# Readers' waits, warming passes and the placing of expert weights in a fused linear attention, soft MoE and gated layer

## The reference

```python
# 1. linear attention with decay; batch 4, heads 8, sequence 768, head size 48
for t in range(S):
    cur = einsum('bhd,bhe->bhde', u[None] * kt, vt)
    y[:, :, t] = einsum('bhd,bhde->bhe', rt, state + cur)
    state = w[None, :, :, None] * state + einsum('bhd,bhe->bhde', kt, vt)
# 2. soft MoE on x of 3072 x 384; 8 experts x 4 slots, hidden 1024
logits = x @ phi
d = softmax over tokens;  slot_input = d.T @ x
h = relu(slot_input[e] @ w1[e]);  slot_out[e] = h @ w2[e]
x = (softmax over slots of logits) @ slot_out
# 3. layer with a gate, d_ff 2048
h = x @ w_in;  g = h * sigmoid(1.702 * h);  out = g @ w_out
```

## Time and profile before

| what | value |
|---|---|
| timed runs, median (lowest to highest) | 395.88 us (395.13 to 398.88) |
| profiled execution: its time | 394.21 us |
| profiled execution: its span | 392.4 us |
| mean granted clock of PE, share of full | 0.982 |
| PE busy | 376.1 us, 96% of the span |
| DVE / ACT / POOL busy | 229.1 / 187.5 / 112.1 us |
| transfers | 63.77 MB, mean 163 GB/s over the span |

### The profile page before, as it was taken

How to read it: one execution, slowest core, us unless ns; L and a number is a source line. 1 busy time by engine, 2 the same in 40 slices (tenths; PEclk the granted TensorE clock), 3 DMA queues, 4 the chain that set the end, 5 groups by cost and what they waited for, 6 DMA issues and landing times.

```text
span 392.4 us, 9064 instructions
## 1 busy us (share of the span) xinstructions
PE 376.1 (96%) x3206; PEld 296.4 (76%) x3206; DVE 229.1 (58%) x419; ACT 187.5 (48%) x432; POOL 112.1 (29%) x125
## 2 busy tenths in 40 slices
PE   4599999999999999899999999999999999999996
PEld 4487787878787444478888888888888888888885
DVE  5477888777885400187665565565565565565561
ACT  1034445555444531376656546544644564555552
POOL 5678987888774020054310000000000000000000
PEclk9579999999999999999999999999999999999999
DMA  7799999999999989930002000200200020002002
GB/s 233 246 364 389 368 381 342 355 345 352 375 326 372 373 287 388 393 121 3 0 0 82 1 0 0 80 0 0 82 0 0 0 80 0 0 0 80 0 2 81
DMA packets 28966, 63.77 MB, mean 163 GB/s; under 512 B 3088, under 2 KB 17056, under 8 KB 28560
## 3 DMA queue, kind: packets, MB, share of 16 engines
q1 hardware_dynamic: 27600, 62.99, 44.4%
q10 hardware_dynamic: 1344, 0.49, 0.7%
HBM read 58.75 MB, written 4.72 MB: 162 GB/s over the span
## 4 chain that ended last, share of the span: by engine, by line
PE 78%; DMA 9%; POOL 5%; SPq 3%; issue 2%; DVE 2%; ACT 0%; DVEq 0%; POOLq 0%
PE bank L592 11%; PE bank L590 11%; PE bank L591 11%; PE pair L590 5%; PE pair L592 5%; PE pair L591 5%; DMA krb<-kr 5%; PE bank L337 4%; PE pair L375 4%; DMA ring<-win 4%; PE bank L577 4%; PE pair L366 3%; PE pair L358 3%; PE bank L396 2%; POOL rkn L1031 2%
## 5 line engine op out<-in xcount | busy, mean ns | idle before, releaser
L813 DVE TENSOR_TENSOR gf<-bank,sg 128x512 f32<-128x512 f32 x72 | 49.7, 692 | 63.4 <-ACT sg L981 63.2
L981 ACT ACTIVATE sg<-bank 128x512 f32<-128x512 f32 x72 | 42.9, 598 | 73.3 <-PE bank L577 73.2
L590 PE MATMUL bank<-glo,whi 128*128 128x512 f32 x192 | 74.7, 389 | 0.0
L592 PE MATMUL bank<-ghi,wlo 128*128 128x512 f32 x192 | 74.7, 389 | 0.0
L591 PE MATMUL bank<-ghi,whi 128*128 128x512 f32 x192 | 74.7, 389 | 0.0
L819 DVE TENSOR_TENSOR glo<-gf,ghi 128x512 fp32r<-128x512 f32 x96 | 69.4, 723 | 0.2
L987 ACT ACTIVATE ghi<-gf 128x512 fp32r<-128x512 f32 x96 | 59.9, 624 | 1.0 <-DVE gf L813 0.9
L591 PEld LDWEIGHTS bank<-ghi,whi 128*128 128x128 f32 x192 | 36.0, 188 | 7.5
L592 PEld LDWEIGHTS bank<-ghi,wlo 128*128 128x128 f32 x192 | 36.0, 188 | 7.5
L590 PEld LDWEIGHTS bank<-glo,whi 128*128 128x128 f32 x192 | 36.0, 188 | 7.5
L861 ACT ACTIVATE yt<-pair 112x512 f32<-112x512 f32 x24 | 14.4, 598 | 56.9 <-PE pair L375 56.9
(11 more groups left out here) (162 smaller groups left out, 520.8 us busy)
## 6 DMA issues: line engine op xcount, KB each, us to landing
ring<-w SPq DMA_DIRECT2D x24, 512.0 KB, 6.2
rkb<-rk SPq DMA_DIRECT2D x23, 512.0 KB, 5.4
krb<-kr SPq DMA_DIRECT2D x24, 384.0 KB, 5.5
ring<-w SPq DMA_DIRECT2D x4, 1536.0 KB, 14.2
ring<-w SPq DMA_DIRECT2D x8, 768.0 KB, 10.6
vb<-v SPq DMA_DIRECT2D x24, 192.0 KB, 5.4
out<-ob SPq DMA_DIRECT2D x18, 256.0 KB, 2.1
ring<-win SPq DMA_DIRECT2D x3, 1024.0 KB, 14.1
```

Of the source, the lines that this page charges most:

```text
L590: pe.matmul(o, w_hi, lo, start=(f == 0), stop=False)
L592: pe.matmul(o, w_lo, hi, start=False, stop=(f == KF - 1)).then_inc(prod_ps, 1)
L813: dve.tensor_tensor(gf[:, f % 2, :], bank[f % 4][:, :], sg[:, f % 2, :], ALU.mult).then_inc(gf_ok, 1)
L981: act.activation(sg[:, f % 2, :], bank[f % 4][:, :], ACT.Sigmoid, scale=1.702).then_inc(sg_ok, 1)
```

## The change

There are five edits. The warming products at the start become 17 in place of 12, and four more stand behind the turning of `wks`. PE's wait for `phi` moves to the last step of the first chunk (step 3). The waits for the constants and the cleared tiles move to their first readers: on DVE to the first `mask`, on POOL to the multiplication by u (constants) and to the first `vd` (cleared tiles). In the order of work, DVE scales step 1 ahead of masking step 0, and POOL makes `kk` of step 0 ahead of the bonus of step 1. SP loads no w1 in the first chunk, five pieces in each of chunks 1 to 4 (two of them in the last step of a chunk), and four in the last chunk; there are 24 pieces in both kernels.

```diff
-WARM = 12
+WARM = 17
@@ SP, step
-                sp.dma_start(ring_flat[:, bass.ds(n * FE, FE)], w1_v[n]).then_inc(w1_in, 16)
+                if not is_first(c):
+                    for i in (b,) if b < B - 1 or is_last(c) else (b, b + 1):
+                        piece = (B + 1) * (c - 1) + i
+                        sp.dma_start(ring_flat[:, bass.ds(piece * FE, FE)], w1_v[piece]).then_inc(w1_in, 16)
@@ PE, scores and step
                     last.then_inc(wkn_ps, 1)
+                    keep_warm(LG, 4)
...
+                if is_first(c, b - 3):
+                    pe.wait_ge(s_phi, 16 * 5)
...
-            pe.wait_ge(s_phi, 16 * 5)
@@ DVE, ahead of the steps, mask and step
-            dve.wait_ge(zeroed, 5)
-            dve.wait_ge(s_const, 16 * 2)
...
+                if is_first(c, b):
+                    dve.wait_ge(zeroed, 5)
+                    dve.wait_ge(s_const, 16 * 2)
...
-                if not is_first(c, b):
+                if is_first(c, b - 1):
+                    scale(c, b)
                     mask(*prev(c, b))
-                scale(c, b)
+                elif is_first(c, b):
+                    scale(c, b)
+                else:
+                    mask(*prev(c, b))
+                    scale(c, b)
@@ POOL, ahead of the steps, bonus, bonus_values and step
-            pool.wait_ge(s_const, 16 * 2)
-            pool.wait_ge(zeroed, 5)
...
                 pool.wait_ge(rk_ok, n + 1)
+                if is_first(c, b):
+                    pool.wait_ge(s_const, 16 * 2)
...
                 wait(pool, rs_used, n - 1)
+                if is_first(c, b):
+                    pool.wait_ge(zeroed, 5)
...
             def step(c, b):
-                bonus(c, b)
                 if b == 1 and is_first(c):
                     scaled_keys(0, 0)
+                bonus(c, b)
```

## The result

The changed kernel takes 389.28 us (median of four runs, 388.57 to 389.61). The kernel before, timed beside it and in the runs shown ahead, has a median of 396.75 us in four (395.13 to 398.88). The ratio on record is 0.9844, with a 95% interval of 0.981 to 0.9877: faster by 1.2 to 1.9% (the plain ratio of the two medians is 0.981, the interval's lower end). The profiled executions took 394.21 and 389.61 us, 4.6 us apart; the medians are 7.5 us apart.

The account below looks back on a forecast made before the run. PE's work was taken to bound everything from 54 us, moving as a block with its entry to chunk 1. 5.0 us gained there and 0 later gave a median of 390.9 us, range 389.0 to 394.0.

Parts of the forecast that it names:

- The start: Chunk 0 up to scores 4: earlier waits, new order and no w1 bring scores 4 from 31.41 to 26.4, gaining 5.0 us.
- the warming term: PE's start: ten more products at 0.196 us an instruction take 1.96 us more, so warming ends at 9.5.
- more is gained: Rival, chance 0.07: at the start kk begins at 11.4 and another microsecond comes free, giving 389.5 us.
- A clock of 1.00 from 10 to 24 us: Sign to look for in the changed profile: PE's clock stays at full level through the start.
- The rival had the fall: Rival, chance 0.15: PE's clock falls again near 13 us, about 2.1 us reach scores 3, result 393.0 us.
- The step that puts four more warming products behind the turning: PE between 11.2 and 12.8: 8 instructions, 1.0 to 1.6 us, fill idle time before scores 1; cover thin by 0.4.
- So 0 is my value: Fifth w1 piece in chunks 1 to 4: costs 0 us, with ends at 0 and 5.2 us.
- the estimate of 399.4 us: Chunks 1 to 4 at the skill's 341 GB/s: four chunks 8.5 us longer; the prediction held the trace against it.
- The slack of 4.0 us: Seventh vd ready at 42.95, its reader starts at 46.99; taken as room for loads delayed by the fifth piece.
- the queue has no spare room: Rival, chance 0.12: each fifth piece in chunks 1 to 4 adds 1.3 us, 5.2 us in all, result 396.1 us.
- The tail moved as a block: Last chunk and w_in load: shift with the entry, PE's wait for w_in stays 1.6 us; one backlogged piece would cost 1.3.
- The sum: Whole kernel: 5.0 us gained at the entry to chunk 1, 0 later; profiled execution 389.2 us, median 390.9 us.

Follow-up runs that it names:

- the second execution: The changed kernel run again unchanged; its profiled execution took 390.79 us, median 389.71 us, ratio 0.9826 to the kernel before.
- phi_as_before: The changed kernel with PE's wait for phi ahead of all steps again; 392.61 us, ratio 0.9947 to the kernel before.
- order_as_before: The changed kernel with the old order of work on POOL and DVE; 391.16 us, ratio 0.9898 to the kernel before.
- bridge_both: The changed kernel with 12 warming products at the start, 13 behind the turning, 6 behind the state of step 0; 389.17 us, ratio 0.9816.
- warm_as_before: The changed kernel with 12 warming products at the start and without the four behind the turning; 389.08 us, ratio 0.9825 to the kernel before.
- bridge_none_step4: bridge_both with w1 pieces 0, 1, 1, 2 by step in chunk 1 and five in each later chunk; 388.58 us, ratio 0.9804.
- w1_only: The kernel before with only the new placing of w1; 393.13 us, ratio 0.9921.
- w1_as_before: The changed kernel with w1 loaded one piece in each step as before; 391.62 us, ratio 0.9895 to the kernel before.

## Why the prediction was right, and where it was not

**The start: right, each stage up to 0.9 us earlier than forecast.** Forecast and measured: scores 0 at 9.5 and 8.66; first `kk` 11.8 and 11.35; third `krb` issued 12.9 and 12.38; scores 1 13.2 and 12.98; scores 2 18.25 and 17.58; scores 4 26.4 and 25.84. The gain at the entry was 5.57 us against 5.0. Some 0.4 us of the difference is the warming term: it was taken at 0.196 us an instruction, and 34 of them took 5.91 us in this execution, 0.174 each (they came faster towards the end: the row of 5 to 6 us has 7 and that of 7 to 8 us has 11, both with a granted clock of 1.00). In the second execution they took 6.79, 0.200 each, with scores 0 at 9.51 and `kk` at 11.81, as forecast, scores 1 and 2 at 12.94 and 17.99, 0.3 us early, and scores 4 at 27.12, 0.7 late behind the fall of the clock. phi_as_before and order_as_before show the mechanism, the wait for `phi` and POOL's order acting through the first `kk`. The rival "more is gained" had asked for a `kk` at 11.4, and it was at 11.35 in the first execution.

**"A clock of 1.00 from 10 to 24 us": wrong.** It fell in both executions. The rival had the fall and priced it at 2.1 us. At 13.6 it costs next to nothing, as DVE waits for POOL's product (14.41) and not for scores 1: bridge_both, whose clock did not fall, entered chunk 1 only 0.17 us earlier. At 18.8 it costs 0.8 us at the entry. So the mechanism of the rival was there and its price was that of the wrong place. The step that puts four more warming products behind the turning, as cover for the clock, also fails: it fell with them, and warm_as_before has neither them nor the five, and is as fast.

**"So 0 is my value" for the fifth piece: right for chunks 2 to 4, wrong for chunk 1.** The loop ran at 386 GB/s with chunks 18.64 us apart, and the estimate of 399.4 us did not come. The Trainium skill ("DMA: Bandwidth & Descriptors", Bandwidth) gives its 341 GB/s for transfers of 1 MB issued from GpSimd; here SP's queue moved more than that with loads of 192 to 512 KB. Chunk 1 lost 1.10 us. The slack of 4.0 us was read from `vd`, but the wait that ended last went another way: a late `krb` of step 7 holds up POOL, then DVE's `dds`, and behind `dds` stand mask 7 and scaling 8 in DVE's order, for which PE waits (1.18 us ahead of scores 8). In the changed kernel:

```profile
38.78 1.01 POOL L1041 TENSOR_TENSOR rkn<-krb 128x384 f32<-128x384 f32 x1 [0.92 <-DMA krb<-kr]
...
40.90 0.55 DVE L676 TENSOR_REDUCE dds<-rkn 128x8 f32<-128x384 f32 x1 [1.52 <-POOL rkn L1046]
...
43.16 1.36 DVE L688 COPY_PREDICATED at<-keep,bank 128x512 f32<-128x512 int32 x2 [0.31 <-issue]
...
44.41 1.27 DVE L669 TENSOR_TENSOR rks<-rkb,bank 112x512 f32<-112x512 f32 x2
```

That `krb` took 6.5 us from issue to landing, against 5.2 for the same step before:

```profile
krb<-kr SPq DMA_DIRECT2D x1, 384.0 KB, 6.5
```

```profile
krb<-kr SPq DMA_DIRECT2D x1, 384.0 KB, 5.2
```

Over chunk 1 the queue gave 396 GB/s at a share of 1.03, close to the 403 that the prediction took for full. The rival "the queue has no spare room" was right for this one chunk, with 1.1 of its 5.2 us. So the term that failed is the 0 for what the w1 pieces cost behind the earlier entry: it measured 1.1 us. And it is not the fifth piece itself that costs them, since bridge_none_step4 has two pieces in step 7 as well and loses nothing; the backlog was there by step 5.

**The tail moved as a block: right** to 0.1 us in this execution; in the second the last chunk took 0.8 us more.

**The sum.** 5.57 - 1.10 + 0.1 = 4.6 us between the profiled executions, where 5.0 was forecast. That they are so near is in part luck, as the entry was 0.6 us better than forecast and chunk 1 cost 1.1 us that the sum had at 0. The forecast for the median, 390.9, is 1.6 us too high, and the measured 389.28 lies 0.3 us inside the range. The forecast moved the median by the gain of one execution, and the medians lie further apart. The kernel before is itself spread: in the two groups with the widest spread its runs at a mean granted clock of 0.974 to 0.979 took 397.1 to 399.3 us, those at 0.986 or 0.987 took 393.5 to 396.6. A mean of 0.974 over 396 us is some 20 us at the lower level ((1 - 0.974) x 396 / 0.5), 0.987 is 10; its profiled execution, at 0.982 and 394.21 us, was faster than most. But those at 0.981 to 0.983 in the same two groups took 395.1 to 397.1 us, up to 2.9 us more than that execution at nearly the same mean clock, so the clock does not account for all of the spread. The changed kernel's runs are at 0.991 to 0.999 and within 388.4 to 390.8 us. So the change also takes away most of the time at the lower level, and with it the runs in which the kernel before is slowest, which a sum over one execution can't show. That this makes up the rest of the difference between the medians is likely and not shown. Nor is it shown which edit does it. w1_only keeps 0.983 to 0.987, while phi_as_before (17 products, early wait) has 0.990 to 0.996 and warm_as_before (12 products, late wait) 0.991 to 0.996. The length of the idle gap does not settle it: w1_only was idle for 3.82 us ahead of scores 0 and then at the lower level for 10.24 us, warm_as_before for 3.79 us ahead of scores 1 and then for 3.42. The other edits, which these two kernels have and w1_only has not, may have a part in it.

Left open: why the queue gave 241 to 299 GB/s in stretches between 10 and 22 us at shares of 0.78 to 0.90, and 386 to 396 later at 1.01 to 1.03 (w1_as_before, with w1 in the first chunk, had 393 from 14.06 to 20.89), what sets the size of chunk 1's loss beside the entry, and why the last chunk took 16.81 us in one execution of the changed kernel and 17.60 in the other.

## What to carry to other kernels

A wait belongs at its reader, and the step to look for behind it is the first one that issues the next load: here the first `kk`, through which two of the edits act, so that their gains should not simply be added. When loads are moved out of a crowded stretch, ask what stands in the queue in the stretch that now comes earlier, and measure slack on each path from a landing to the bounding engine, in the order of the engine between them. Where a start depends on when the clock changes, look at two executions before pricing it: the entry to chunk 1 differed by 1.3 us between two of the same kernel.

## What was not expected of the hardware

The stretch at the lower clock was 3.41 us long and began at 13.57 in one execution of the changed kernel and at 18.78 in another; the warming products took 5.91 and 6.79 us. In the Trainium skill, "TensorE: Matmul & The Clock Gate" (What's actually happening) says that the point of the change varies from run to run with where the kernel's start falls. That it varies, these two executions show; the reason, no run here shows. Before those two falls PE had idled for 1.72 us ahead of scores 1 and for 1.95 us ahead of scores 2; the prediction had held a fall unlikely (0.15). In bridge_both and bridge_none_step4, where the longest gap between the first product and 26 us was 0.98 us, the clock did not fall, and it did not fall behind the 1.16 us ahead of scores 8 in bridge_both either. In order_as_before and w1_as_before the stretch was 6.83 us long and began at 12.62 and at 14.06.
